# Sparse attention and a gated MLP on one core: the gate's layer norm on other engines, in a new instruction order

## What is computed

```python
h = x @ w_in
c = np.float32(np.sqrt(2.0 / np.pi))
h = 0.5 * h * (1.0 + np.tanh(c * (h + 0.044715 * h ** 3)))
u, v = (h[..., :d_ff // 2].copy(), h[..., d_ff // 2:].copy())
mu = np.mean(v, axis=-1, keepdims=True)
var = np.mean((v - mu) ** 2, axis=-1, keepdims=True)
v_n = (v - mu) / np.sqrt(var + 1e-06) * g_ln
v_s = np.einsum('ts,bsd->btd', w_sg, v_n) + b_sg[None, :, None]
gated = u * v_s
return (x + gated @ w_out).astype(np.float32)
```

## Time and profile before

| what | value |
|---|---|
| median of 3 runs | 230.11 us (229.93 to 230.97) |
| the profiled execution's own time | 230.35 us |
| its span, first to last instruction | 228.3 us |
| busy, share of the span: PE, DVE, ACT, POOL | 205.7 us (90%), 186.5 us (82%), 167.2 us (73%), 121.9 us (53%) |
| chain that ended last: PE, DVE, POOL, ACT, issue | 58%, 23%, 8%, 7%, 3% |
| mean granted clock of PE, share of full speed | 0.96 |

### The profile page before, as it was taken

One profiled execution on the slowest core, in us unless ns is written; L12 is line 12 of the kernel. 1 busy time (PEld: TensorE's weight loads), 2 busy tenths in 40 slices (PEclk: granted clock), 3 DMA queues, 4 the chain that ended last, 5 costly groups with the idle time before them and its releaser, 6 DMA issues.

```text
span 228.3 us, 5988 instructions
## 1 busy us (share of the span) xinstructions
PE 205.7 (90%) x2367; PEld 133.0 (58%) x2381; DVE 186.5 (82%) x535; ACT 167.2 (73%) x250; POOL 121.9 (53%) x157
## 2 busy tenths in 40 slices
PE   7899999999639999989993399999999999999993
PEld 3466777666327667667561157768744667745551
DVE  3999998899708999999995068897698885977994
ACT  3879999998934899998789029898877898456000
POOL 8406967964996548496369915538725014106000
PEclk9999999999958999999999569999999999999998
DMA  7999999999991956948998029895793003000307
GB/s 156 249 219 207 208 266 369 293 209 248 226 220 37 210 118 173 229 86 122 257 217 188 0 46 124 176 236 129 120 217 80 3 0 139 5 0 0 138 16 262
DMA packets 97515, 35.39 MB, mean 155 GB/s; under 512 B 92112, under 2 KB 92880, under 8 KB 97488
## 3 DMA queue, kind: packets, MB, share of 16 engines
q1 hardware_dynamic: 97056, 34.61, 69.4%
q10 hardware_dynamic: 432, 0.39, 0.5%
HBM read 24.77 MB, written 6.29 MB: 136 GB/s over the span
## 4 chain that ended last, share of the span: by engine, by line
PE 58%; DVE 23%; POOL 8%; ACT 7%; issue 3%; DVEq 0%
PE PSG L963 15%; POOL vhat L934 8%; PE PSC L779 8%; PE PSG L982 7%; PE PSG L946 5%; PE PSG L857 5%; PE PSG L525 5%; PE PSG L906 4%; DVE Wall L564 3%; DVE stats L915 3%; ACT E L785 3%; DVE Bn L581 2%; DVE XS L874 2%; DVE m L730 2%; PE PSC L359 2%
## 5 line engine op out<-in xcount | busy, mean ns | idle before, releaser
L785 ACT ACTIVATE E<-PSC 128x1024 bf16<-128x1024 f32 (+1 forms) x72 | 62.6, 917 | 14.4 <-PE PSC L779 13.4
L963 PE MATMUL PSG<-wsgT,vhat 128*128 128x384 bf16 x192 | 38.2, 350 | 12.7 <-POOL vhat L934 12.7
L790 POOL TENSOR_SCALAR_AFFINE_SELECT E<-E 128x768 bf16<-128x768 bf16 x24 | 21.0, 883 | 32.4 <-ACT E L785 32.2
L779 PE MATMUL PSC<-QA,KA 128*128 128x128 bf16 (+2 forms) x336 | 37.2, 247 | 0.0
L969 DVE SCALAR_TENSOR_TENSOR PSG<-PSG,glnT,bsgbc 128x384 f32<-128x384 f32 x32 | 19.6, 621 | 18.5 <-PE PSG L963 18.1
L963 PEld LDWEIGHTS PSG<-wsgT,vhat 128*128 128x128 bf16 x192 | 19.1, 104 | 25.8 <-issue 16.2
L779 PEld LDWEIGHTS PSC<-QA,KA 128*128 128x128 bf16 x336 | 23.8, 98 | 9.7 <-ACT E L785 3.1
L946 PE MATMUL PSG<-xT,winb 128*128 128x384 bf16 x128 | 23.9, 327 | 0.1
L438 POOL CAST QA<-qT 64x768 bf16<-64x768 f32 (+1 forms) x23 | 19.4, 843 | 8.7 <-ACT qT L435 6.9
L564 DVE TENSOR_REDUCE Wall<-PSG 128x12 f32<-128x384 f32 x40 | 20.6, 545 | 3.2 <-PE PSG L525 2.9
L906 PE MATMUL PSG<-winb,xT 128*128 128x512 bf16 x91 | 22.1, 379 | 0.8 <-ACT vgb L910 0.3
(11 more groups left out here) (111 smaller groups left out, 389.2 us busy)
## 6 DMA issues: line engine op xcount, KB each, us to landing
qn<-in_q_dram SPq DMA_DIRECT2D x32, 192.0 KB, 4.5
vn<-in_v_dram SPq DMA_DIRECT2D x16, 384.0 KB, 5.3
out_dram<-osb SPq DMA_DIRECT2D x21, 256.0 KB, 2.5
kn<-in_k_dram SPq DMA_DIRECT2D x20, 192.0 KB, 4.9
kn<-in_k_dram SPq DMA_DIRECT2D x6, 384.0 KB, 5.5
uT<-in_moe_w_sg_dram SPq DMA_DIRECT2D x4, 384.0 KB, 4.9
vgb<-in_moe_w_in_dram SPq DMA_DIRECT2D x3, 512.0 KB, 8.2
vhat<-in_moe_w_sg_dram SPq DMA_DIRECT2D x2, 384.0 KB, 5.7
```

Source lines behind the costliest of these rows:

```text
L779: r = e.matmul(t.ap()[:, o:o + n], KA[w][i][:, 128 * kb:128 * kb + 128], QA[w][i][:, q0:q0 + n], start=True, stop=True)
L785: P.op("act", lambda e, t=t, c0=c0, c1=c1, i=i: e.activation(E[es][:, i, c0:c1], t.ap()[:, 0:c1 - c0], ACTF.Exp, scale=SCALE), act(c1 - c0 ...
L790: P.op("pool", lambda g, ev=ev: g.affine_select(ev, ev, pattern=[[0, NT], [1, 128]], compare_op=ALU.is_ge, fill=0.0, base=0, channel_multi ...
L963: r = e.matmul(t.ap()[:, 0:TG], vhat[s][:, sb, 128 * fb:128 * fb + 128], wsgT[:, sb, TG * tg:TG * tg + TG], start=(sb == 0), stop=(sb == N ...
```

## The change

The table is written anew: order of all five queues, PSUM slots, engine choices. The engine list that the planner has for `vhat` loses POOL.

```diff
-            o.alts = {"act": (704, 809), "dve": (456, 548), "pool": (590, 640)}
+            o.alts = {"act": (704, 809), "dve": (456, 548)}
...
     "pe": (
-        "1 49 50 58 60 83 65 141 84 139 94 92 206 196 107 106 99 198 200 115 117 174 202 204 163 172 164 252 258 "
...
+        "1 50 49 58 60 83 65 139 141 84 94 92 206 196 107 106 99 198 200 115 117 164 163 204 202 222 252 122 258 "
...
     "filler": (
         "49:8 58:2 83:2 "),
     "engine": (
...
-        "xev_3_2:dve xev_3_3:dve vhat_0_4:pool vhat_0_5:pool vhat_0_0:pool vhat_0_1:pool vhat_1_4:pool "
-        "vhat_1_0:pool vhat_1_3:pool vhat_1_5:pool vhat_1_1:pool vhat_3_2:pool "),
...
+        "kev_5_0_1:dve wev_0_0:dve xev_0_1:dve xev_0_3:dve kev_5_1_1:dve kev_5_1_0:dve wev_3_1:dve vhat_0_4:dve "
+        "vhat_0_3:dve vhat_0_5:dve vhat_0_2:dve vhat_0_0:dve qd_4_1:dve kev_6_0_1:dve qev_15_0:dve qd_13_0:dve "
```

More of the change, by code:

```diff
@@ L1079 @@
     "pe": (
[15 rows of a table removed]
-    "act": (
[10 rows of a table removed]
-    "dve": (
[17 rows of a table removed]
-    "pool": (
[13 rows of a table removed]
[15 rows of a table added]
+    "act": (
[10 rows of a table added]
+    "dve": (
[17 rows of a table added]
+    "pool": (
[13 rows of a table added]
     "slots": (
[L1139 to L1142, removed]
+        "10232321301330001100011010132022101100231010000010123132101110010132010001010103201001013223322332322322"
+        "22323333323211011022000110000023111001101000321011101032011001232323233322232333222232332301100132010011"
+        "11230110011101102310000101230101013232232223333232232232323332001110321101110330011100321101010320100310"
+        "1201202313022303110321"),
     "filler": (
@@ L1145 @@
     "engine": (
[10 rows of a table removed]
+        "mrow_1_1_0:act qcast_0:act mrow_0_1_0:act wic_3:act rel_5:act qcast_4_1:act rel_6:act rel_7:act "
+        "qcast_7_1:act rel_9:act rel_8:act rel_10:act rel_11:act rel_12:act rel_13:act vhat_1_5:act "
+        "kcast_13_1:act kcast_14_1:act qd_11_1:act qd_11_0:act qd_12_1:act kcast_15_0:act vhat_3_5:act "
+        "vhat_3_3:act st_3_1:act st_3_5_256:act st_3_3_256:act kev_0_1:dve kev_2_1:dve kev_2_0:dve kev_3_1:dve "
+        "kev_4_0_1:dve kev_4_0_0:dve qev_4_1:dve qev_5_0:dve wev_0_1:dve kev_4_1_1:dve kev_5_0_0:dve "
+        "kev_5_0_1:dve wev_0_0:dve xev_0_1:dve xev_0_3:dve kev_5_1_1:dve kev_5_1_0:dve wev_3_1:dve vhat_0_4:dve "
+        "vhat_0_3:dve vhat_0_5:dve vhat_0_2:dve vhat_0_0:dve qd_4_1:dve kev_6_0_1:dve qev_15_0:dve qd_13_0:dve "
+        "xev_3_0:dve xev_3_1:dve xev_3_3:dve "),
 }
```

## The result

The changed kernel takes **215.93 us** (median of 4 runs, 214.51 to 216.57) against 230.54 us (229.93 to 231.1) for the kernel before beside it: a ratio of 0.936, interval 0.930 to 0.942.

The account below looks back on a forecast made before the run. PE was taken as the bound, idle 12.7 us for POOL's normalisations and then at half clock. 230.35 + 1.5 - 5.6 - 9.0 = 217.25, less 0.24 for the median: 217.0 us, range 211 to 223.

Parts of the forecast that it names:

- The mechanism and the sum: Whole kernel: PE's two waits for POOL's normalisations and the half clock behind them go; 217.0 us.
- Batch 1: Third stage, nmr1 to nmr2: PE's wait and half clock go, ScalarE limits the gain; -9.0 us, bounds -6 and -10.3.
- Batch 0: Second stage, nmr0 to nmr1: PE's wait and half clock go, VectorE limits the gain; -5.6 us, bounds -3.5 and -7.3.
- all of PE's loss comes back: Rival, batches 0 and 1: VectorE's and ScalarE's bounds are soft, PE regains everything; 212.0 us, chance 0.16.
- The start: Up to nmr0: dummies between the key halves +2.5, fewer VectorE copies -1.0; net +1.5 us, bounds -0.5 and +3.
- What costs nothing: Batches 2 and 3: VectorE already normalises batch 2, and PE hides batch 3's new split; 0 us.
- VectorE and POOL at the same time: Batches 0 and 1: five VectorE normalisations beside POOL casts take 2.4 to 3.4 us; the sum takes 2.4.
- VectorE and POOL collide: Rival, batches 0 and 1: each normalisation waits for a POOL cast; 224.4 us if all collide, 221 if half; chance 0.12.
- the new order makes waits of its own: Rival, all rewritten queues: late masks or casts give back a third of the 14.6 us; 222 us, chance 0.15.
- The slower rival: First stage: PE's clock stays low after the dummies move; 239 us if through the whole stage, chance 0.04.

Follow-up runs that it names:

- the normalisations alone: Kernel before with only its ten POOL normalisations put on VectorE, directly behind their nmr: 218.47 us, ratio 0.947.
- the clock's part alone: Kernel before with 28 and 40 dummy matmuls on PE during its two waits for POOL: 225.99 us, ratio 0.980.
- the dummies ahead: Changed kernel with all eight start dummies put back ahead of the first half of the keys' transposition: 213.1 us, ratio 0.924.
- the quiet run: Changed kernel, eight dummies ahead of the first keys, POOL's next instruction held until the last of VectorE's five normalisations in batches 0 and 1: 212.77 us.
- batch 0 alone: Kernel before with only batch 0's four POOL normalisations put on VectorE: 224.53 us.
- batch 1 alone: Kernel before with only batch 1's five POOL normalisations put on VectorE: 225.08 us.
- the loud run: Changed kernel, eight dummies ahead of the first keys, four extra unread POOL copies of 128x512 behind rstd of batches 0 and 1: 215.1 us.

## Why the prediction was right, point by point

**The mechanism and the sum** (217.0, measured 215.93, inside 211 to 223). The runs show each link: the normalisations alone make 12 us of the gain, the clock's part alone 4.6, and the two batches nearly add up. The forecast was that of the likeliest case. What held less well are the reasons for what is left of each stage.

**Batch 1** (-9.0, measured -9.2). The third stage is 48.0 us, as forecast. That ScalarE is what keeps it from the 10.3 us of PE's loss isn't shown: ScalarE is busy 40.76 of 48.0 us and waits for PE's score tiles again (0.55 us above), while PE is busy 46.80 and 40 us of the chain in that stage lie on it.

**Batch 0** (-5.6, measured -6.8). VectorE was taken as the bound of that stage with 52.0 + 1.0 busy and 2.1 idle. With the old order and only batch 0 moved it is the fullest engine there: the stage is 55.16, VectorE is busy for 54.03 of it and PE for 52.06, and of the chain that ended last 26 us of that stage lie on VectorE, 18 on PE. With the new order this no longer holds: VectorE is busy 52.65 of 54.0, PE 52.86, and 33 us of the chain lie on PE, 12.5 on VectorE. VectorE's added work is 0.7 and not 1.0, and of its idleness 1.35 is left, not 2.1. So the last 1.2 us belong to the order, and the stage is nearer to PE's own -7.3 than to the bound that the sum took. This is the rival "all of PE's loss comes back" by a part; that VectorE's idle times move with the order was the doubt named there.

**The start** (+1.5, measured +0.7 in one execution). Executions scatter here by about 1 us, so I compare all with the same start. With the old start `nmr0` ends at 57.71, 57.14, 57.42, 58.49 and 58.25 us, mean 57.80; with the new order and the dummies ahead at 56.37, 57.05 and 56.97, mean 56.80; with the change's start at 58.44, 59.60 and 59.36, mean 59.13. So the new order without the dummies gave 1.0, what was forecast for the copies alone, and the dummies cost 2.3, forecast 2.5. The terms named for that 2.5 (0.85, 1.7 or 3.4, less 0.9) add up to 1.65 or 3.35 and not to 1.0 or 2.8; the eight dummies took 3.00 us, since most of them ran at half clock. That VectorE carries the first stage isn't shown either. Ahead of the first `nmr` PE was as busy (49.65 and 49.7 of 52.1 us), and the chain before has 26 us on PE and 24 on VectorE there, in the changed kernel 41 and 4.

**What costs nothing.** Behind `nmr2` there is 0.35 us of difference. Batch 3's split is hidden by PE, as said.

**VectorE and POOL at the same time: this step failed.** The sum took 2.4 us, the lower end of its 2.4 to 3.4, for five normalisations because "fewer and shorter things run beside"; they took 2.9 in both batches, and PE's cover of 0.1 to 0.4 us did not hide it: 0.40 and 0.53 us of waiting are left, and the quiet run gets rid of them. The argument behind it was wrong. It read from batch 3 that VectorE's four don't all come behind POOL's normalisation, and took that against the exclusive lock. Two of the four did get in while it ran, but the last ended 0.28 us behind its end (211.51 and 211.23), and POOL's normalisation is no fair witness for POOL's casts. In the changed kernel batch 0's first three normalisations take 0.72 us each and end 0.28 us behind the ends of a cast and two memsets, and batch 1's third meets one cast:

```profile
113.21 0.95 POOL L438 CAST vx<-vn 128x768 bf16<-128x768 f32 x1 [1.22 <-DMA vn<-in_v_dram]
```

That normalisation begins at 113.39 and takes 1.05 us, the longest of the ten, and ends 0.28 us behind the end of the cast; the other four, with nothing or only the cast's beginning beside them, take 0.53 to 0.55. The same 0.28 us lies between the end of a POOL instruction and that of the normalisation that came second in the runs with batch 0 alone, with batch 1 alone and with the dummies ahead. The Trainium skill ("SBUF — State Buffer", section "Who interferes with whom") says just this: of a POOL instruction and a VectorE operation that uses the ports shared with it, whichever issues first has them for its whole instruction. For casts, copies and memsets the runs agree with it, against the prediction; for POOL's own normalisation they don't, since in batch 3 two of VectorE's four got in while one POOL instruction ran.

**The rival "VectorE and POOL collide"** was priced at 0.84 us for each of five, 4.2 us a batch. With POOL busy without a gap in the loud run it is 1.3 us: a normalisation only waits for what is left of one POOL instruction, since the two alternate there. The copies of that run are shorter than the rival's casts (0.61 and 0.84 us), so its price isn't tested in full; the changed kernel has one cast and two memsets beside batch 0 and one cast beside batch 1. Nor does a wait always end with the first POOL instruction. With the dummies ahead, VectorE's fourth normalisation of batch 0 met a cast at its start and came in only behind the memset that followed (it ends at 59.02, the memset at 58.74), 1.25 us long; VectorE's and POOL's timelines there:

```profile
57.77 1.25 DVE L934 TENSOR_SCALAR vhat<-vgb,mv,rstd 128x512 bf16<-128x512 f32 x1
```

```profile
57.78 0.61 POOL L438 CAST woutb<-osb 128x512 bf16<-128x512 f32 x1 [1.96 <-DMA osb<-in_moe_w_out_dram]
58.33 1.05 POOL L755 MEMSET QA<- 64x384 uint32 x2
```

**The rival "the new order makes waits of its own"** did not come true with the normalisations on VectorE: behind the start no wait of PE for another releaser sums to over 0.8 us, as before. It did with them on POOL, by a wait that the prediction had not on its list. It was in the trace of before, though: the same subtraction, twice, 0.75 us at 23.64 and 0.94 as below, with the cast that it stood behind.

```profile
36.60 0.94 DVE L574 TENSOR_TENSOR Wall<-Wall 128x24 f32<-128x24 f32 x1
```

```profile
36.46 1.04 POOL L438 CAST winb<-xT 128x1024 bf16<-128x1024 f32 x1 [0.92 <-DMA xT<-in_moe_w_in_dram]
```

It ends at 37.54, the cast at 37.50; undisturbed it takes 0.17 us. The same section of the Trainium skill names it: a VectorE instruction with two inputs in SBUF contends with a POOL instruction that reads SBUF.

**The slower rival** (the clock doesn't rise at the start) is out: from 7.8 us on the dummies' own pace is the full one, and the clock row reads 9 in every slice. What the prediction says of the kernel before, full clock from 1.24 us on, is too early: its nine dummies came every 0.43 us, the pace of the low level.

## What to carry to other kernels

A row of slow instructions on one engine, all of which one consumer needs, costs its length and then the consumer's climb back to full clock; here the second part was 4.6 of 17 us, and dummy matmuls bought it back without touching the cause. When VectorE takes over work, look at what POOL has beside it and hold POOL's casts back if they can wait; a row of POOL casts can stretch a VectorE instruction of 128 x 24 to 2.9 us. An order written for one placement of the work is not good in itself: the same order was worth 2.5 us with the normalisations on VectorE and cost 6.4 with them on POOL, 3.7 of which hung on one cast that came 0.7 us too early for the subtraction beside it.

## What the runs showed of the hardware that was not expected

- VectorE's normalisations and POOL's copies alternate instruction by instruction in the loud run, where both have a row: a pitch of 0.75 us on each, against 0.46 us for VectorE alone. POOL pays too: its cast of 128 x 512 took 0.80 us beside them and 0.61 in the quiet run.
- The subtraction with two SBUF inputs was let in behind the first of two POOL instructions in one place (0.75 us at 23.64 in the kernel before, a cast with a causal cut directly behind it) and only behind the fourth of five in another (2.88 us). What decides that stays open; it wasn't tried.
- POOL's own normalisation (2.1 to 2.4 us an instruction) does not shut VectorE out for its length: beside the one of batch 3 in the kernel before, four on VectorE took 0.55, 0.92, 0.53 and 0.94 us; the second and third ended while it ran, the fourth 0.28 us behind it.
- At the start the clock row reads 1.00 while the dummies of the changed kernel still follow each other every 0.43 us; from 7.8 us on the same dummies come every 0.22. The first record of the granted clock in that trace begins at 7.60 us (5.18 in the kernel before), so the 1.00 ahead of it is no reading.
